# Attention visits in a fused matmul stream: TensorE's waits gathered at the head of each visit

## The chip, the cores and the metric

The kernel runs on one core of a Trainium2 chip. The metric is the time of one execution on the device in microseconds (us). Before the change it is 863.22 us, the median of three runs from 862.84 to 863.50 us.

## What is computed

A gated linear attention over 4 batches, 8 heads, 768 tokens and 48 channels per head, followed by two dense two-layer blocks over the 3072 tokens (model width 384, hidden width 2048). Cut to what matters:

```python
for t in range(S):
    state = alpha[:, :, t, :, None] * state + np.einsum('bhd,bhe->bhde', k[:, :, t], v[:, :, t])
    y[:, :, t] = np.einsum('bhd,bhde->bhe', q[:, :, t], state)
x = np.ascontiguousarray(y.transpose(0, 2, 1, 3)).reshape(B * S, H * D)
h = x @ w_in;   x = (h * np.clip(h + 3.0, 0.0, 6.0) / 6.0) @ w_out      # first block
h = x @ w_in2;  out = np.maximum(h, 0.0) ** 2 @ w_out2                  # second block
```

## The kernel before

**Steps.** TensorE's program is one list of 192 steps and two more to drain. Step g computes one slice of 128 hidden channels for 512 tokens: `hidden(g)` (L1027) is 9 matmuls of 128x512, and `project(g - 2)` (L1040) is 9 matmuls that use the slice of two steps earlier. Both split each fp32 operand into a high and a low part, so three products are summed. In between, ScalarE makes the gate (L572) and rounds the high part (L580), VectorE multiplies (L761), and GpSimd (POOL) subtracts to get the low part (`low(g)`, L499). Steps 0 to 95 are the first dense block, 96 to 191 the second.

**Attention.** The first 128 tokens of each batch (tiles 0 to 3) are done before step 0. The rest is cut into 20 tiles, 4 to 23, one tile being 64 tokens of two batches. Their TensorE work is put between the steps, in a **visit** per tile. A visit for tile t comes after the two matmul groups of its step and consists of

1. `carry_straight(t)` (L921): 8 small matmuls (L916) of the state with the queries, after its waits;
2. `attend(t)` (L960): 16 small matmuls (L969) of masked scores with values;
3. for t from 5 to 22, `add_up(t - 1)` (L986): 16 small matmuls (L995) of keys with values, for the state;
4. for t from 8 to 22, `score_later(t + 1)` (L883): 16 small matmuls (L900) of keys with queries of the **next** tile;
5. `carry_crossed(t)` (L930): 8 more matmuls (L916) of state with queries.

The profile counts each small matmul as two. From tile 9 on, the scores of a tile are thus made in the visit of the tile before (`with_output` is true); I call the visits of tiles 8 to 22 the **15 fused visits**. For tiles 4 to 8 the score is made by itself one or more steps ahead of the tile's own visit. The steps of the visits stand in `ATTEND_AT` and `LATER_ATTEND_AT`: steps 4, 7, 10, 13 of the first sixteen, then 1, 5, 9, 13 of each sixteen.

**What feeds a visit.** For a tile, VectorE scans the decays (L676, L684), and then POOL multiplies the keys (L489, `scale_keys`) and the queries (L494, `scale_queries`) by them. The semaphore `q_scaled` counts finished query scalings. In POOL's program this pair stands right behind `low(g)` of the step g that `scaled_at` names; for tiles 9 to 23 that is the step just before the fused visit in which they are scored. SyncE loads values (`v_loaded`) and, by way of device memory, the turned keys (L401, `keys_loaded`). VectorE masks the scores (`masked`) and multiplies the state (`state_decayed`), and the vector and scalar engines take the output y out of PSUM (`x_hi`, `x_lo`). TensorE itself counts `attended` after a visit's `attend`, `u_made` after `add_up`, and `y_made` after `carry_crossed`.

Of the kernel before, what the change touches and what calls it, by code (L numbers as in the profile page):

```python
# [12 lines left out]
BATCH, HEADS, SEQ, HD = 4, 8, 768, 48  # L13
# [9 lines left out]
TILES = CHUNKS * BATCH  # L23
# [46 lines left out]
LAST_SUMMED = TILES - 3  # L70
# [14 lines left out]
def slot_of(t):  # L85

    return t if t < BATCH else BATCH + t % 2


def turn_of(t):  # L90

    return 1 if t < BATCH else (t - BATCH) // 2 + 1
# [13 lines left out]
def with_output(t):  # L106

    return t - BATCH >= len(FIRST_SCORE_AT)
# [14 lines left out]
def tiles_at(g, step_of):  # L123
    return [t for t in range(BATCH, TILES) if step_of(t) == g]


def hi_parts(t):


    return t + 1 if t < BATCH - 1 else BATCH - 1 + KT + 2 * (t - BATCH + 1)  # L130


def pieces_of(t):

    return 2 * (t + 1) if t < BATCH else 2 * BATCH + t - BATCH + 1
# [22 lines left out]
def chunked_program(nc, block, semaphores, att_in, v_first, v_in, w_in1, w_out1, w_in2, w_out2, out, out_of_range,  # L158
# [4 lines left out]
    with ExitStack() as ctx:  # L163
# [12 lines left out]
        def sem(name):  # L176
            return semaphores.enter_context(nc.semaphore(name))
# [67 lines left out]
        def keys(t):  # L245
            return pairs(slot(t)[0:ROWS, 0:PAIRS * TILE])

        def queries(t):
            return pairs(slot(t)[0:ROWS, PAIRS * TILE:KQ_W])

        def values(t):
            return inputs[:, t % 2, SLOT_W:SLOT_W + DM]
# [11 lines left out]
        def side_of(j, parity):  # L264

            return parity ^ j % 2
# [31 lines left out]
        def half_rows(half):  # L298
            return slice(HALF * half, HALF * half + HD)
# [14 lines left out]
        v_loaded = [sem(f"v_loaded{i}") for i in range(BATCH + 2)]  # L314
# [9 lines left out]
        k_scaled = sem("k_scaled")  # L324
        q_scaled = sem("q_scaled")
# [5 lines left out]
        masked = sem("masked")  # L331
        blocks_turned = sem("blocks_turned")
        turned_stored = sem("turned_stored")
        keys_loaded = sem("keys_loaded")
# [6 lines left out]
        x_hi = sem("x_hi")  # L341
        x_lo = sem("x_lo")
# [14 lines left out]
        def wait_loaded(engine, semaphores, t):  # L357
            engine.wait_ge(semaphores[slot_of(t)], 16 * turn_of(t))
# [9 lines left out]
        def load_flag(name, engine):  # L368
            engine.wait_ge(range_judged, 3)
            flags[name] = engine.value_load(out_of_range[0:1, 0:1], min_val=0, max_val=1)  # L370
# [491 lines left out]
        def _(pe):  # L862
# [18 lines left out]
                                last.then_inc(scored, 1)  # L881

            def score_later(t):  # L883
                pe.wait_ge(k_scaled, t + 1)
                pe.wait_ge(q_scaled, t + 1)
                pe.wait_ge(masked, pieces_of(t - 1))
                if with_output(t):
                    pe.wait_ge(attended, t - BATCH)
                else:
                    pe.wait_ge(y_made, t)  # L890
                    pe.wait_ge(x_hi, hi_parts(t - 1))
                    pe.wait_ge(x_lo, hi_parts(t - 1))
                    pe.wait_ge(state_made, pieces_of(max(t - 2, BATCH - 1)))
                for j in range(PAIRS):
                    for b in range(2):
                        cols = slice(PART * b, PART * (b + 1))
                        for parity in range(2):
                            rows = half_rows(parity)
                            place = SCORE_COLS[parity] + j * PART
                            last = nc.tensor.matmul(att_all[cols, place:place + PART], keys(t)[rows, j, cols],  # L900
                                                    queries(t)[rows, j, cols], start=parity == 0 or not with_output(t),
                                                    stop=True, skip_group_check=True)
                last.then_inc(scored, 1)

            def carry_on(t, crossed):

                for j in range(0, PAIRS, 2):
                    for side in range(2):  # L910
                        for parity in range(2):
                            batch = parity ^ crossed
                            pair = j + (parity ^ side)
                            rows = half_rows(parity)
                            place = OUTPUT_COLS[batch] + pair * PART
                            last = nc.tensor.matmul(att_all[half_rows(side), place:place + PART],  # L916
                                                    state[rows, t % 2 * 2 + batch, pair, :],
                                                    queries(t)[rows, pair, PART * batch:PART * (batch + 1)],
                                                    start=not crossed and j == 0, stop=True, skip_group_check=True)
                return last  # L920

            def carry_straight(t):

                pe.wait_ge(state_decayed, t - BATCH + 1)
                pe.wait_ge(masked, pieces_of(t))
                pe.wait_ge(q_scaled, t + 1)
                pe.wait_ge(x_hi, hi_parts(t - 1))
                pe.wait_ge(x_lo, hi_parts(t - 1))
                carry_on(t, 0)

            def carry_crossed(t):
                pe.wait_ge(attended, t - BATCH + 1)
                if BATCH < t <= LAST_SUMMED + 1:
                    pe.wait_ge(u_made, t)
                carry_on(t, 1).then_inc(y_made, 1)
# [22 lines left out]
                last.then_inc(y_made, 1)  # L958

            def attend(t):  # L960
                wait_loaded(pe, v_loaded, t)
                pe.wait_ge(masked, pieces_of(t))
                for j in range(PAIRS):
                    for parity in range(2):
                        head = 2 * j + parity
                        for b in range(2):
                            tokens = slice(PART * b, PART * (b + 1))
                            place = OUTPUT_COLS[b] + j * PART
                            last = nc.tensor.matmul(att_all[half_rows(side_of(j, parity)), place:place + PART],  # L969
                                                    values(t)[tokens, head * HD:(head + 1) * HD], masked_part[tokens, parity, j, :],  # L970
                                                    start=False, stop=True, skip_group_check=True)
                last.then_inc(attended, 1)
# [11 lines left out]
                last.then_inc(u_made, 1)  # L984

            def add_up(t):  # L986
                pe.wait_ge(keys_loaded, 16 * (t - BATCH + 1))
                wait_loaded(pe, v_loaded, t)
                for j in range(PAIRS):
                    for parity in range(2):  # L990
                        head = 2 * j + parity
                        for b in range(2):
                            tokens = slice(PART * b, PART * (b + 1))
                            place = SUM_COLS[b] + j * HD
                            last = nc.tensor.matmul(att_all[half_rows(parity), place:place + HD],  # L995
                                                    k_tok[tokens, j, HD * parity:HD * (parity + 1)],
                                                    values(t)[tokens, head * HD:(head + 1) * HD], start=b == 0, stop=True,
                                                    skip_group_check=True)
                last.then_inc(u_made, 1)
# [86 lines left out]
            for g in range(2 * STEPS + LAG):  # L1086
                if g < 2 * STEPS:
                    hidden(g)
                if g >= LAG:
                    project(g - LAG)  # L1090
                for t in tiles_at(g, attend_at):
                    carry_straight(t)
                    attend(t)
                    if BATCH < t <= LAST_SUMMED + 1:
                        add_up(t - 1)
                for t in tiles_at(g, score_at):
                    score_later(t)
                for t in tiles_at(g, attend_at):
                    carry_crossed(t)
                if g == 2 * STEPS + LAG - 1:  # L1100
                    load_flag("pe", pe)
                if g == STEPS - FT + 8:
                    pe.wait_ge(range_judged, 2)
                    nc.tensor.matmul(att_ps[0][0:1, 0:1], in_range_all, causal[0:ROWS, TILE - 1:TILE], start=True, stop=True).then_inc(range_counted, 1)
# [290 lines left out]
```

## Time and profile before

| | |
|---|---|
| Median of three runs | 863.22 us |
| The profiled execution, as timed | 862.91 us |
| Its span in the profile | 861.2 us |
| TensorE matmul busy in the span | 853.0 us (99%) |
| VectorE, ScalarE, POOL busy | 38%, 38%, 37% |
| TensorE's granted clock, mean | 0.999 |

The profiled execution is 0.31 us below the median of the runs. The page's busy lines and the chain of waits tell which engine sets the time. The rows of the timeline give start and length of a merged group of instructions. Matmuls are pipelined, so consecutive groups overlap in the timeline: a group's length runs to the end of its last matmul, and the start of that last matmul is the group's end less the length of a single one.

### The profile page before, as it was taken

To read this page: it belongs to the slowest core of one execution; us is meant where nothing else is said; L and a number is where in the kernel's file an instruction comes from. 1 tells how busy PE (TensorE), PEld (TensorE's weight loads), DVE (VectorE), ACT (ScalarE), POOL (GpSimd) and SP (SyncE) were. 2 spreads that over 40 slices of the span, in tenths; PEclk is the share of its full clock that TensorE was granted. 3 is DMA by queue.
4 is the path that set the end of the run, shared out by engine and by line. 5 is a ranking of instruction groups with operands and counts; after the bars stand their busy time and mean duration, and the time that the engine had idled before them with its cause. 6 is when DMAs were issued, how large, how long until landed. Compare 5 with 4: busy or idle time off the path is not lost.

```text
span 861.2 us, 15383 instructions
## 1 busy us (share of the span) xinstructions
PE 853.0 (99%) x6312; PEld 705.5 (82%) x6312; DVE 330.7 (38%) x466; ACT 328.8 (38%) x586; POOL 315.3 (37%) x248
## 2 busy tenths in 40 slices
PE   8999999999999999999999999999999999999998
PEld 7877788888888888888888888888888888888886
DVE  8886545565445556422334312211211211211111
ACT  4754443343333333333454423333333323333332
POOL 2754443433443334432333333333323333333332
PEclk9999999999999999999999999999999999999999
DMA  9633323233223332200323000000000100100101
GB/s 351 260 105 92 79 72 108 73 89 79 71 71 95 85 89 76 64 16 6 108 76 111 1 0 21 17 1 8 29 1 0 37 1 1 37 0 1 37 1 38
DMA packets 67495, 51.84 MB, mean 60 GB/s; under 512 B 50784, under 2 KB 57184, under 8 KB 67424
## 3 DMA queue, kind: packets, MB, share of 16 engines
q1 hardware_dynamic: 67424, 50.84, 19.3%
q8 instruction: 51, 0.84, 0.4%
q14 instruction: 20, 0.16, 0.1%
HBM read 40.60 MB, written 8.26 MB: 57 GB/s over the span
## 4 chain that ended last, share of the span: by engine, by line
PE 96%; DMA 1%; issue 1%; ACT 0%; SPq 0%; POOL 0%; DVE 0%; ACTq 0%; DVEq 0%
PE h_ps L1027 46%; PE o_ps L1040 45%; PE att_all L916 1%; PE att_all L900 1%; DMA w_in_raw<-w_in 1%; PE att_all L969 1%; PE att_all L995 1%; SPq L379 0%; PE h_ps L953 0%; POOL g_parts L499 0%; DVE inputs L676 0%; POOL inputs L494 0%; POOL inputs L489 0%; ACT k_tok L538 0%; DVE x_mid L715 0%
## 5 line engine op out<-in xcount | busy, mean ns | idle before, releaser
L499 POOL TENSOR_TENSOR g_parts<-h_act,g_parts 128x512 fp32r<-128x512 f32 x192 | 257.0, 1339 | 523.9 <-ACT g_parts L580 523.9
L1040 PE MATMUL o_ps<-g_parts,w_out_hi 128*128 128x512 f32 x1152 | 327.1, 389 | 0.0
L1027 PE MATMUL h_ps<-x_parts,w_in_hi 128*128 128x512 f32 x1152 | 295.9, 392 | 0.0
L1040 PEld LDWEIGHTS o_ps<-g_parts,w_out_hi 128*128 128x128 f32 x1152 | 216.3, 188 | 45.0
L1027 PEld LDWEIGHTS h_ps<-x_parts,w_in_hi 128*128 128x128 f32 x1152 | 214.2, 188 | 45.3
L580 ACT ACTIVATE g_parts<-h_act 128x512 fp32r<-128x512 f32 x192 | 121.4, 632 | 268.2 <-PE o_ps L1040 241.9
L764 DVE SCALAR_TENSOR_TENSOR h_act<-h_ps,h_gate 128x512 f32<-128x512 f32 x96 | 66.4, 691 | 290.5 <-ACT h_gate L575 290.5
L1040 PE MATMUL o_ps<-g_parts,w_out_lo 128*128 128x512 f32 x576 | 165.6, 389 | 0.0
L1027 PE MATMUL h_ps<-x_parts,w_in_lo 128*128 128x512 f32 x576 | 161.9, 389 | 0.0
L1027 PEld LDWEIGHTS h_ps<-x_parts,w_in_lo 128*128 128x128 f32 x576 | 108.1, 188 | 22.7
L1040 PEld LDWEIGHTS o_ps<-g_parts,w_out_lo 128*128 128x128 f32 x576 | 108.1, 188 | 22.4
L761 DVE SCALAR_TENSOR_TENSOR h_act<-h_gate,h_ps 128x512 f32<-128x512 f32 x96 | 65.4, 681 | 139.7 <-ACT h_gate L572 139.6
L572 ACT ACTIVATE h_gate<-h_ps 128x512 f32<-128x512 f32 x96 | 57.4, 598 | 116.6 <-PE h_ps L1027 116.5
L575 ACT ACTIVATE h_gate<-h_ps 128x512 f32<-128x512 f32 x96 | 57.4, 598 | 110.8 <-PE h_ps L1027 110.8
L684 DVE TENSOR_TENSOR_SCAN inputs<-inputs,seeds 112x520 f32<-112x520 f32 x20 | 37.4, 1872 | 0.7
L742 DVE TENSOR_TENSOR tails<-att_all,tails 112x128 fp32r<-112x128 f32 x20 | 5.9, 293 | 57.8 <-ACT x_parts L559 57.8
L676 DVE TENSOR_TENSOR_SCAN inputs<-inputs,seeds 112x520 f32<-112x520 f32 x20 | 25.6, 1280 | 2.5 <-DVE seeds L673 0.5
L494 POOL TENSOR_TENSOR inputs<-inputs 112x512 f32<-112x512 f32 x20 | 24.5, 1226 | 0.0
L489 POOL TENSOR_TENSOR inputs<-inputs 112x512 f32<-112x512 f32 x20 | 23.9, 1196 | 0.0
L715 DVE STREAM_TRANSPOSE x_mid<-inputs 128x512 f32<-128x512 f32 x18 | 19.7, 1092 | 0.0
L916 PEld LDWEIGHTS att_all<-inputs,state 48*48 48x48 f32 x640 | 12.5, 120 | 8.4 <-issue 7.9
L916 PE MATMUL att_all<-inputs,state 48*48 48x64 f32 x640 | 17.5, 222 | 0.8 <-PE att_all L995 0.6
(107 smaller groups left out, 357.8 us busy)
## 6 DMA issues: line engine op xcount, KB each, us to landing
inputs<-att_in SPq DMA_DIRECT2D x20, 772.0 KB, 4.5
w_in_raw<-w_in SPq DMA_DIRECT2D x8, 768.0 KB, 7.7
w_out_raw<-w_out SPq DMA_DIRECT2D x8, 768.0 KB, 9.2
result<-inputs SPq DMA_DIRECT2D x18, 256.0 KB, 2.3
inputs<-v_in SPq DMA_DIRECT2D x20, 192.0 KB, 2.8
k_tok<-turned_keys SPq DMA_DIRECT2D x18, 192.0 KB, 2.9
turned_keys<-x_mid SPq DMA_DIRECT2D x36, 64.0 KB, 2.3
x_parts<-tails SPq DMA_DIRECT2D x120, 16.0 KB, 2.1
```

Of the source, the lines that this page charges most:

```text
L494: nc.gpsimd.tensor_tensor(by_chunk(t, queries(t)), by_chunk(t, queries(t)), to_token(t)[:, :, 0:chunk(t)], ALU.mult).then_inc(q_scaled, 1)
L499: nc.gpsimd.tensor_tensor(g_parts[:, g % 2, 1, :], h_act[:, g % 2, :], g_parts[:, g % 2, 0, :].bitcast(F32), ALU.subtract).then_inc(g_lo, 1)
L572: nc.scalar.activation(h_gate[:, g % 2, :], h_ps[g % 2][:, :], ACT.Relu, bias=0.5, scale=1.0 / 6.0).then_inc(gate_made, 1)
L575: nc.scalar.activation(h_gate[:, g % 2, :], h_ps[g % 2][:, :], ACT.Relu).then_inc(gate_made, 1)
L580: nc.scalar.activation(g_parts[:, g % 2, 0, :], h_act[:, g % 2, :], ACT.Copy).then_inc(g_hi, 1)
L676: nc.vector.tensor_tensor_scan(scanned(t, ATT_W), scanned(t, KQ_W), other_seeds(t), 0.0, ALU.mult, ALU.max).then_inc(from_end_made, 1)
L684: nc.vector.tensor_tensor_scan(loaded[:, ::-1], loaded[:, ::-1], other_seeds(t), 0.0, ALU.mult, ALU.max).then_inc(to_token_made, 1)
L761: nc.vector.scalar_tensor_tensor(h_act[:, g % 2, :], h_gate[:, g % 2, :], 1.0, h_ps[g % 2][:, :], ALU.min, ALU.mult).then_inc(act_made, 1)
L764: nc.vector.scalar_tensor_tensor(h_act[:, g % 2, :], h_ps[g % 2][:, :], 0.0, h_gate[:, g % 2, :], ALU.max, ALU.mult).then_inc(act_made, 1)
L916: last = nc.tensor.matmul(att_all[half_rows(side), place:place + PART], state[rows, t % 2 * 2 + batch, pair, :], queries(t)[rows, pair, PA ...
L1027: last = nc.tensor.matmul(h_ps[g % 2][:, :], w[:, m, cols], x_parts[:, n % 2, part, m, :], start=m == 0 and i == 0, stop=m == KT - 1 and i ...
L1040: return nc.tensor.matmul(o_ps[m][:, :], w[:, f, m * P:(m + 1) * P], g_parts[:, g % 2, part, :], start=f == 0 and w is w_out_hi and part = ...
```

## The change

Four functions of TensorE's program change; no computation, buffer or transfer does, and no other engine's program does.

- `wait_for_visit(t)` takes the place of the waits of `carry_straight(t)`. It waits for `state_decayed` and `masked` as before, no longer for `q_scaled` of its own tile, `x_hi` and `x_lo`, and in addition for `v_loaded`, for `keys_loaded` (where an `add_up` follows) and, where a `score_later(t + 1)` follows in the visit, for `q_scaled` of tile t + 1.
- `attend` and `add_up` have no waits of their own any more.
- `score_later(t)` no longer waits for `k_scaled` and `masked`; in the fused visits it waits for `attended` alone. Standing alone (tiles 4 to 8) it keeps `q_scaled`, `y_made`, `x_hi`, `x_lo` and `state_made`.
- `carry_crossed` keeps its waits for `attended` and `u_made`.

```diff
             def score_later(t):
-                pe.wait_ge(k_scaled, t + 1)
-                pe.wait_ge(q_scaled, t + 1)
-                pe.wait_ge(masked, pieces_of(t - 1))
+
                 if with_output(t):
                     pe.wait_ge(attended, t - BATCH)
                 else:
+                    pe.wait_ge(q_scaled, t + 1)
                     pe.wait_ge(y_made, t)
...
-            def carry_straight(t):
+            def wait_for_visit(t):
+
 
                 pe.wait_ge(state_decayed, t - BATCH + 1)
                 pe.wait_ge(masked, pieces_of(t))
-                pe.wait_ge(q_scaled, t + 1)
-                pe.wait_ge(x_hi, hi_parts(t - 1))
-                pe.wait_ge(x_lo, hi_parts(t - 1))
-                carry_on(t, 0)
+                wait_loaded(pe, v_loaded, t)
+                if BATCH < t <= LAST_SUMMED + 1:
+                    pe.wait_ge(keys_loaded, 16 * (t - BATCH))
+                if t + 1 < TILES and with_output(t + 1):
+                    pe.wait_ge(q_scaled, t + 2)
...
             def attend(t):
-                wait_loaded(pe, v_loaded, t)
-                pe.wait_ge(masked, pieces_of(t))
...
             def add_up(t):
-                pe.wait_ge(keys_loaded, 16 * (t - BATCH + 1))
-                wait_loaded(pe, v_loaded, t)
...
                 for t in tiles_at(g, attend_at):
-                    carry_straight(t)
+                    wait_for_visit(t)
+                    carry_on(t, 0)
                     attend(t)
```

The first place is TensorE's program at the first fused visit, that of tile 8. In brackets stand the semaphores for which an instruction waits, with `L` the line that issues it. Before:

```order
L916 MATMUL att_all<-inputs,state 48x64 [waits x_hi,q_scaled,x_lo,masked,state_decayed]
L916 MATMUL att_all<-inputs,state 48x64 x7
L969 MATMUL att_all<-masked_t,inputs 48x64 [waits masked,v_loaded4]
L969 MATMUL att_all<-masked_t,inputs 48x64 x15
L995 MATMUL att_all<-inputs,k_tok 48x48 [waits v_loaded5,keys_loaded]
L995 MATMUL att_all<-inputs,k_tok 48x48 x15
L900 MATMUL att_all<-inputs 64x64 [waits masked,attended,q_scaled,k_scaled]
L900 MATMUL att_all<-inputs 64x64 x15
L916 MATMUL att_all<-inputs,state 48x64 [waits u_made,attended]
```

The same visit after the change (line numbers differ by up to 3):

```order
L915 MATMUL att_all<-inputs,state 48x64 [waits keys_loaded,v_loaded4,q_scaled,masked,state_decayed]
L915 MATMUL att_all<-inputs,state 48x64 x7
L968 MATMUL att_all<-masked_t,inputs 48x64 x16
L992 MATMUL att_all<-inputs,k_tok 48x48 x16
L899 MATMUL att_all<-inputs 64x64 [waits attended]
L899 MATMUL att_all<-inputs 64x64 x15
L915 MATMUL att_all<-inputs,state 48x64 [waits u_made,attended]
```

No matmul moved. The wait for the next tile's `q_scaled` stood in front of the fourth group and now stands in front of the first; of the ten waits inside the visit three are left (`attended` twice and `u_made`), and the head has five as before.

The second place is TensorE's program at the visit of tile 5, which has no score in it. Before:

```order
L916 MATMUL att_all<-inputs,state 48x64 [waits x_hi,q_scaled,x_lo,masked,state_decayed]
L916 MATMUL att_all<-inputs,state 48x64 x7
L969 MATMUL att_all<-masked_t,inputs 48x64 [waits masked,v_loaded5]
L969 MATMUL att_all<-masked_t,inputs 48x64 x15
L995 MATMUL att_all<-inputs,k_tok 48x48 [waits v_loaded4,keys_loaded]
L995 MATMUL att_all<-inputs,k_tok 48x48 x15
L916 MATMUL att_all<-inputs,state 48x64 [waits u_made,attended]
```

After the change:

```order
L915 MATMUL att_all<-inputs,state 48x64 [waits v_loaded5,keys_loaded,masked,state_decayed]
L915 MATMUL att_all<-inputs,state 48x64 x7
L968 MATMUL att_all<-masked_t,inputs 48x64 x16
L992 MATMUL att_all<-inputs,k_tok 48x48 x16
L915 MATMUL att_all<-inputs,state 48x64 [waits u_made,attended]
```

Here the two loads are waited for at the head, and `q_scaled` not at all. POOL's program is the same before and after.

## Rows read from the trace of the kernel before

**Rows 1.** The page: header, busy time by engine, granted clock, chain by line.

```profile
span 861.2 us, 15383 instructions
...
PE 853.0 (99%) x6312; PEld 705.5 (82%) x6312; DVE 330.7 (38%) x466; ACT 328.8 (38%) x586; POOL 315.3 (37%) x248
...
PEclk9999999999999999999999999999999999999999
```

**Rows 2.** Waits of TensorE: engine, line, releaser: us in total, times, longest us.

```profile
PE h_ps L865 <- POOL causal L472: 2.0, 1, 2.0
PE o_ps L953 <- DVE h_gate L722: 0.7, 1, 0.7
PE att_all L916 <- PE att_all L995: 0.6, 3, 0.2
...
PE att_all L983 <- ACT k_tok L538: 0.3, 1, 0.3
```

**Rows 3.** Timeline, PE, fused visit of tile 9: start us, length us, instructions merged.

```profile
125.45 0.84 PE L1040 MATMUL o_ps<-g_parts,w_out_hi 128*128 128x512 f32 x3
126.22 0.44 PE L916 MATMUL att_all<-inputs,state 48*48 48x64 f32 x16
126.49 0.63 PE L969 MATMUL att_all<-masked_t,inputs 64*48 64x64 f32 x32
126.93 0.54 PE L995 MATMUL att_all<-inputs,k_tok 64*48 64x48 f32 x32
127.41 0.69 PE L900 MATMUL att_all<-inputs 48*64 48x64 f32 x32
127.90 0.43 PE L916 MATMUL att_all<-inputs,state 48*48 48x64 f32 x16
```

**Rows 4.** Groups by line, PE: busy us, mean ns of one, idle before.

```profile
L969 PE MATMUL att_all<-masked_t,inputs 64*48 64x64 f32 x640 | 12.6, 216 | 0.0
L995 PE MATMUL att_all<-inputs,k_tok 64*48 64x48 f32 x576 | 9.7, 205 | 0.0
```

**Rows 5.** Timeline, PE, fused visit of tile 8.

```profile
107.44 0.44 PE L916 MATMUL att_all<-inputs,state 48*48 48x64 f32 x16
...
108.16 0.54 PE L995 MATMUL att_all<-inputs,k_tok 64*48 64x48 f32 x32
108.79 0.69 PE L900 MATMUL att_all<-inputs 48*64 48x64 f32 x32
```

**Rows 6.** Timeline, PE, fused visit of tile 22, the last.

```profile
367.58 0.44 PE L916 MATMUL att_all<-inputs,state 48*48 48x64 f32 x16
...
368.29 0.54 PE L995 MATMUL att_all<-inputs,k_tok 64*48 64x48 f32 x32
368.74 0.69 PE L900 MATMUL att_all<-inputs 48*64 48x64 f32 x32
```

**Rows 7.** Timeline, POOL, around the visit of tile 9.

```profile
123.02 1.29 POOL L499 TENSOR_TENSOR g_parts<-h_act,g_parts 128x512 fp32r<-128x512 f32 x1 [1.60 <-ACT g_parts L580]
124.27 1.19 POOL L489 TENSOR_TENSOR inputs<-inputs 112x512 f32<-112x512 f32 x1
125.42 1.19 POOL L494 TENSOR_TENSOR inputs<-inputs 112x512 f32<-112x512 f32 x1
127.10 1.27 POOL L499 TENSOR_TENSOR g_parts<-h_act,g_parts 128x512 fp32r<-128x512 f32 x1 [0.49 <-ACT g_parts L580]
```

**Rows 8.** Timeline, POOL, query scaling around the visit of tile 8.

```profile
107.50 1.19 POOL L494 TENSOR_TENSOR inputs<-inputs 112x512 f32<-112x512 f32 x1
```

**Rows 9.** Timeline, POOL, around the visit of tile 22.

```profile
364.38 1.29 POOL L499 TENSOR_TENSOR g_parts<-h_act,g_parts 128x512 fp32r<-128x512 f32 x1 [2.79 <-ACT g_parts L580]
...
366.77 1.20 POOL L494 TENSOR_TENSOR inputs<-inputs 112x512 f32<-112x512 f32 x1
```

**Rows 10.** Timeline, PE, the visit of tile 4: no add_up and no score in it.

```profile
43.53 0.63 PE L969 MATMUL att_all<-masked_t,inputs 64*48 64x64 f32 x32
44.27 0.44 PE L916 MATMUL att_all<-inputs,state 48*48 48x64 f32 x16
```

**Rows 11.** Timeline, SyncE's queue: a load of keys (L401), one of values (L389).

```profile
51.72 0.57 SPq L401 DMA_DIRECT2D k_tok<-turned_keys  x1
...
66.93 0.62 SPq L389 DMA_DIRECT2D inputs<-v_in  x1
```

**Rows 12.** The page, DMA issues: instructions, KB each, median us from issue to landing.

```profile
inputs<-v_in SPq DMA_DIRECT2D x20, 192.0 KB, 2.8
...
k_tok<-turned_keys SPq DMA_DIRECT2D x18, 192.0 KB, 2.9
```

**Rows 13.** Timeline, PE, first group of the visits of tiles 5 and 6.

```profile
57.97 0.44 PE L916 MATMUL att_all<-inputs,state 48*48 48x64 f32 x16
...
73.08 0.44 PE L916 MATMUL att_all<-inputs,state 48*48 48x64 f32 x16
```

**Rows 14.** Busy table of 12 to 20 us: us, busy PE, PEld, DVE, ACT, POOL, PEclk.

```profile
12.00:20.00 8.00, 7.34 (x159) 6.68 (x155) 7.64 (x13) 5.24 (x12) 1.19 (x1) 1.00 1.03 410
```

**Rows 15.** Timeline, PE, in that stretch: in brackets the idle time before and its releaser.

```profile
16.41 1.53 PE L953 MATMUL o_ps<-h_gate,first_v 128*64 128x128 f32 x24 [0.66 <-DVE h_gate L722]
```

**Rows 16.** The chain that ended last: one group of each kind in a step.

```profile
345.00 2.04 PE h_ps L1027 x9
347.04 2.04 PE o_ps L1040 x9
```

## Prediction

> **What bounds the kernel now.** I read the page first. TensorE is busy 99% of the span and the other compute engines under 40% each, at a granted clock near full in every slice [rows 1]. So whatever TensorE waits for at one place is added to the time, and whatever it saves comes off it. The view of waits then says that TensorE hardly waits for anybody: five small rows near the start and in the first block, and none that names `x_hi`, `x_lo`, `k_scaled`, values or loaded keys in a visit [rows 2]. Taking waits away can therefore give back only the cost of passing a wait that is already satisfied, and for that one has to look at the seams between groups in the timeline.
>
> The timeline of a fused visit shows the seams [rows 3]. The start of a group's last matmul is its end less one matmul, 0.216 us for L969 and 0.205 us for L995 [rows 4]. L969 ends at 126.49 + 0.63 = 127.12, so its last matmul starts at 126.90, and L995 follows at 126.93: a seam of 0.03 us. L995's last matmul starts at 126.93 + 0.54 - 0.205 = 127.27, and L900, the score, starts at 127.41: a seam of 0.14 us. The last seam, L900 to L916, has L916 start at 127.90 while L900 ends at 128.10, an overlap of a whole matmul. Only the seam in front of the score, with its four waits, costs anything.
>
> The third thing to read is when the awaited events happen. The one that matters is the scaling of the next tile's queries on POOL, because its wait moves from the fourth group to the first. For tile 9's visit POOL's L494 ends at 125.42 + 1.19 = 126.61 [rows 7], but the visit starts at 126.22 and its score at 127.41 [rows 3]. **The scaling ends inside the visit**: soon enough for where the wait stands now, and 0.39 us too late for the head.
>
> **The change part by part.**
>
> *The moved wait, 14 visits.* In tile 22's visit it is the same: L494 ends at 366.77 + 1.20 = 367.97 [rows 9], the head is at 367.58 [rows 6], 0.39 us. These are the first and the last of 14 visits (tiles 9 to 22) with L494 ending 0.38 to 0.40 us behind the head. To this comes the time from POOL's end to TensorE's first matmul. Tile 8 shows it: there L494 ends at 107.50 + 1.19 = 108.69 [rows 8] and the score starts at 108.79 [rows 5], and its other releasers are long done, so 0.10 us. Each of the 14 heads moves back by 0.39 + 0.10 = 0.49 us: 14 x 0.49 = 6.86 us.
>
> *The moved wait, tile 8.* The head is at 107.44 [rows 5] and could now start at 108.79: 1.35 us.
>
> *Do the delays catch up?* I say no. POOL's pair of scalings stands directly behind `low(g)`, and that one starts when ScalarE delivers, 1.60 us after POOL ran dry at tile 9 and 2.79 us at tile 22 [rows 7, 9]. ScalarE is fed by TensorE's hidden matmuls of that step. So when TensorE is late by some time, POOL's scaling is late by the same, and the next head is again 0.39 us too early. Nothing else stands between TensorE's groups that could shrink.
>
> *Waits taken out in front of the score, 15 visits.* The seam there is 0.14 us at tile 9 and 368.74 - (368.29 + 0.54 - 0.205) = 0.115 us at tile 22 [rows 6], between 0.11 and 0.14 us in all 14. At tile 8 it is 108.79 - (108.16 + 0.54 - 0.205) = 0.295 us, since `q_scaled` came late [rows 5]. I take 0.035 us, the neighbouring seam of L969 to L995, for what is left. Is `attended`, still waited for there, in the way? Tile 4's visit has no `add_up` between: L969's last matmul starts at 43.53 + 0.63 - 0.216 = 43.94 and the dependent L916 at 44.27 [rows 10], so the event needs 0.33 us. In a fused visit `add_up` fills 0.37 us of that and more [rows 3], so it is hidden with about 0.07 us to spare. Saving: 0.26 us at tile 8 and on the mean 0.08 us in the other 14, 1.15 us, together 1.4 us. The bounds are nothing and, were the seams to close as L900 to L916 does, 0.4 us more.
>
> The Trainium skill's page "TensorE: Matmul & The Clock Gate" (Part 1, Architectural detail) gives TensorE a queue 64 deep. By that the sequencer would have passed the score's waits far ahead, nothing would be saved there, and the sum would be 1.4 us higher. The seam of 0.14 us beside one of 0.03 us speaks against it [rows 3], so the trace's value stays in the sum; the page's case is the third rival.
>
> *Waits taken out elsewhere.* `masked` and `v_loaded` in front of L969, `v_loaded` and `keys_loaded` in front of L995: the seams there are already 0.03 us [rows 3], so nothing comes back. `x_hi`, `x_lo` and its own `q_scaled` at the head: no row of the waits names them [rows 2], and the head's five waits stay five, so nothing. The bound from the trace is the score's seam, 0.08 us a visit, if they cost what its waits cost; the five that stay make me leave that out.
>
> *Loads waited for earlier.* `keys_loaded` and `v_loaded` come forward by under 0.8 us. The first key load is issued at 51.72 [rows 11] and lands 2.9 us later [rows 12], at 54.6, against a head at 57.97 [rows 13]. The first values loaded in turn are issued at 66.93 and land at 69.7, against a head at 73.08 [rows 13]. That is over 3 us to spare in the tightest place; 0. What hides them is the distance of four steps; if it were gone, each would cost its lateness as the scaling does.
>
> *Visits of tiles 4 to 7 and 23, scores standing alone:* same seams, 0. The seam for `u_made` at tiles 5 to 7 stays. What waits behind TensorE's head is only TensorE's own next step, and the engines that wait for a visit (VectorE's state update, ScalarE's rounding) get it later with four steps until the next.
>
> **Sum:** 6.86 + 1.35 - 1.41 = 6.8 us. The profiled execution becomes 862.91 + 6.8 = 869.7 us; its median lies 0.31 us above, 863.22 + 6.8 = **870.0 us**, 0.8% slower.
>
> **Rivals.**
>
> *Faster: the head's wait is hidden.* POOL's spans are rough by the page's own account, and if the semaphore rose over 0.4 us before L494's recorded end, the head would wait for nothing and only the saving would be left: 863.22 - 1.4 = 861.8 us. It decides at a lateness that equals the saving, 0.08 us a visit. Against it: at tile 8 the score started just 0.10 us after that end, with nothing else to wait for. 3%.
>
> *No change: the delay is caught up.* If POOL ran on a beat of its own, one delay would cure the next visit's, and only tile 8's 1.35 us less 1.4 us would remain: 863.2 us. Against it: POOL idle behind ScalarE before each pair [rows 7, 9]. 3%.
>
> *Slower still, nothing saved in front of the score:* 6.86 + 1.35 = 8.2 us, 871.4 us. For it: `attended` is still waited for. 8%.
>
> *Slower still, the clock falls.* TensorE stood idle for 0.66 us at 16.41 and the granted clock stayed at 1.00 over that stretch, the 2.4 GHz level [rows 14, 15]; tile 8's gap would be 1.35 us. A step is two groups of 9 matmuls at 2.04 us each [rows 16], 4.1 us; one at the 1.2 GHz level costs 4.1 us more, 874 us. 2%.
>
> **How the numbers follow.** The forecast has 84%; its own range is the lateness of 0.38 to 0.40 us, a releaser's time of 0.07 to 0.13 us, a saving from 0.5 to 1.8 us: 14 x 0.45 + 1.32 - 1.8 = 5.8 us to 14 x 0.53 + 1.38 - 0.5 = 8.3 us, or 869.0 to 871.5. That takes in the third rival's 871.4. The runs before spread by 0.3 us to either side, which I add below: 868.7 to 871.5 us. Outside are the first two rivals, the falling clock and a few in a hundred of the forecast's own. A measurement of this kernel can tell 0.2% (1.7 us) from no change. Faster by more than that: 0.02; within: 0.04; slower: 0.94.
>
> **What would show it.** In the new profile the head's L915 should start 0.10 us behind the end of POOL's L494 in every fused visit and TensorE should be listed as waiting for POOL 15 times, some 0.4 to 0.5 us each and 1.3 us once. The seam L992 to L899 should be 0.03 to 0.04 us. The visits of tiles 4 to 7 and 23 should be as before. The prediction is wrong if L494 shifts against the head, if the head does not wait for it, or if the score's seam stays.

## The result, and the profile after

| | before | after the change |
|---|---|---|
| Median | 862.88 us (6 runs, 862.80 to 863.50) | 870.06 us (6 runs, 869.28 to 870.77) |
| Profiled execution, as timed | 862.91 us | 870.47 us |
| Its span | 861.2 us | 868.8 us |

The ratio of the times is 1.0081, with a 95% interval from 1.0070 to 1.0092: slower by 0.8%, 7.2 us between the medians. The forecast was 870.0 us.

The chain of work that ended last now runs through POOL for a part of the time. Its shares by engine, before and after:

```profile
PE 96%; DMA 1%; issue 1%; ACT 0%; SPq 0%; POOL 0%; DVE 0%; ACTq 0%; DVEq 0%
```

```profile
PE 89%; POOL 6%; ACT 2%; DMA 1%; issue 1%; SPq 0%; DVE 0%; ACTq 0%; DVEq 0%
```

The view of waits of TensorE has a new first row (engine, line, releaser: us in total, times, longest us). It answers to [rows 2].

```profile
PE att_all L915 <- POOL inputs L494: 7.8, 15, 1.3
PE h_ps L865 <- POOL causal L472: 2.0, 1, 2.0
PE o_ps L954 <- DVE h_gate L722: 0.7, 1, 0.7
```

TensorE waits for POOL's query scaling 15 times, once in each fused visit, and the longest of them is tile 8's. The timeline of TensorE around tile 9's visit answers to [rows 3] (start us, length us, instructions merged, in brackets the idle time before and its releaser).

```profile
127.05 0.84 PE L1037 MATMUL o_ps<-g_parts,w_out_hi 128*128 128x512 f32 x3
128.36 0.44 PE L915 MATMUL att_all<-inputs,state 48*48 48x64 f32 x16 [0.46 <-POOL inputs L494]
128.59 0.66 PE L968 MATMUL att_all<-masked_t,inputs 64*48 64x64 f32 x32
129.04 0.56 PE L992 MATMUL att_all<-inputs,k_tok 64*48 64x48 f32 x31
129.39 0.23 PE L899 MATMUL att_all<-inputs 48*64 48x64 f32 x1
...
129.43 0.65 PE L899 MATMUL att_all<-inputs 48*64 48x64 f32 x31
129.87 0.43 PE L915 MATMUL att_all<-inputs,state 48*48 48x64 f32 x16
130.24 1.66 PE L1024 MATMUL h_ps<-x_parts,w_in_hi 128*128 128x512 f32 x6
```

The row of the kernel before to compare the last one with:

```profile
128.26 1.65 PE L1027 MATMUL h_ps<-x_parts,w_in_hi 128*128 128x512 f32 x6
```

Before, the head came 126.22 - 125.45 = 0.77 us behind the start of the last three large matmuls; now it is 128.36 - 127.05 = 1.31 us, 0.54 us later. From the head to the next step's first matmul it was 2.04 us (126.22 to 128.26) and is 1.88 us (128.36 to 130.24), 0.16 us less. Net 0.38 us here. (Tile 9's seam before was a bit wide; in the other visits the net is 0.39 to 0.43 us, but for tile 12's, 0.78 us, with a pause behind it.)

POOL around the same visit, answering to [rows 7]:

```profile
124.62 1.29 POOL L499 TENSOR_TENSOR g_parts<-h_act,g_parts 128x512 fp32r<-128x512 f32 x1 [1.60 <-ACT g_parts L580]
...
127.01 1.20 POOL L494 TENSOR_TENSOR inputs<-inputs 112x512 f32<-112x512 f32 x1
```

POOL's idle time in front of `low(g)` is 1.60 us as before. L494 starts 125.42 - 125.45 = 0.03 us ahead of the large group L1040 in the old trace and 127.01 - 127.05 = 0.04 us ahead of it in the new: POOL has moved with TensorE, and each head is again too early by the same amount. At tile 22 the same holds, after the delays of tiles 8 to 21, with 2.79 us of idle time as in [rows 9]:

```profile
371.59 1.29 POOL L499 TENSOR_TENSOR g_parts<-h_act,g_parts 128x512 fp32r<-128x512 f32 x1 [2.79 <-ACT g_parts L580]
...
373.99 1.20 POOL L494 TENSOR_TENSOR inputs<-inputs 112x512 f32<-112x512 f32 x1
```

And tile 8's visit, answering to [rows 5]:

```profile
107.68 0.39 PE L1037 MATMUL o_ps<-g_parts,w_out_hi 128*128 128x512 f32 x1
109.39 0.44 PE L915 MATMUL att_all<-inputs,state 48*48 48x64 f32 x16 [1.33 <-POOL inputs L494]
```

The visits without a score did not change their shape. Behind tile 12's visit the new trace also has a pause with no releaser, which I come back to at the end (PEld is TensorE's weight loads):

```profile
188.88 0.19 PEld L1024 LDWEIGHTS h_ps<-x_parts,w_in_lo 128*128 128x128 f32 x1 [0.52 <-issue]
```

### The profile page after: what moved, and what is told of

Its sections match the earlier page's. It is cut to its first block, busy times and chain, and to the rows that moved or that the text cites. A ratio compares the mean times of both kernels' runs of the same rounds, so it can differ in the third digit from the quotient of the medians.

```text
span 868.8 us, 15308 instructions
## 1 busy us (share of the span) xinstructions
PE 852.1 (98%) x6312; PEld 703.6 (81%) x6312; DVE 330.2 (38%) x466; ACT 328.5 (38%) x586; POOL 315.0 (36%) x248
## 4 chain that ended last, share of the span: by engine, by line
PE 89%; POOL 6%; ACT 2%; DMA 1%; issue 1%; SPq 0%; DVE 0%; ACTq 0%; DVEq 0%
PE h_ps L1024 42%; PE o_ps L1037 41%; POOL g_parts L499 2%; POOL inputs L494 2%; POOL inputs L489 2%; PE att_all L915 2%; DMA w_in_raw<-w_in 1%; PE att_all L899 1%; ACT g_parts L580 1%; PE att_all L968 1%; PE att_all L992 1%; SPq L379 0%; PE h_ps L954 0%; DVE inputs L676 0%; ACT k_tok L538 0%
## 5 line engine op out<-in xcount | busy, mean ns | idle before, releaser
L494 POOL TENSOR_TENSOR inputs<-inputs 112x512 f32<-112x512 f32 x20 | 24.5, 1226 | 0.0
```

What stands on the lines that cost most here:

```text
L494: nc.gpsimd.tensor_tensor(by_chunk(t, queries(t)), by_chunk(t, queries(t)), to_token(t)[:, :, 0:chunk(t)], ALU.mult).then_inc(q_scaled, 1)
```

## The experiments

The medians below are of 11 runs of each kernel, but for the moved wait alone (4 runs) and the two with another order of the waits (5 each). The kernel before ran beside them: its median was 863.15 us beside the first four kernels (27 runs) and 863.01 us beside the last four (21 runs). The seams of single visits are worked out from the rows shown, which are rounded to 0.01 us.

### The moved wait alone

```diff
                 pe.wait_ge(x_lo, hi_parts(t - 1))
+                if t + 1 < TILES and with_output(t + 1):
+                    pe.wait_ge(q_scaled, t + 2)
                 carry_on(t, 0)
```

> The kernel before, with one wait added: in the 15 fused visits the head also waits for q_scaled of the next tile. All other waits stay. My theory (the moved wait is the whole loss): each of 14 heads moves back to 0.10 to 0.15 us behind the end of POOL's L494, 0.49 to 0.53 us later than now, and tile 8's 1.35 us, while the score's seam keeps its 0.11 us and loses 0.18 us at tile 8: 14 x 0.51 + 1.35 - 0.18 = 8.3 us more than before, about 871.2 us, and 1 us above the changed kernel. Rival (the removed waits or a changed instruction stream cost something as well): clearly under 869 us.

Measured: 872.02 us, ratio 1.0101 (1.0085 to 1.0116), 8.9 us over the kernel before. TensorE's waits, and tile 9's visit in the timeline:

```profile
PE att_all L916 <- POOL inputs L494: 8.0, 15, 1.3
```

```profile
127.12 0.84 PE L1042 MATMUL o_ps<-g_parts,w_out_hi 128*128 128x512 f32 x3
128.44 0.44 PE L916 MATMUL att_all<-inputs,state 48*48 48x64 f32 x16 [0.47 <-POOL inputs L494]
...
129.12 0.56 PE L997 MATMUL att_all<-inputs,k_tok 64*48 64x48 f32 x32
129.59 0.69 PE L900 MATMUL att_all<-inputs 48*64 48x64 f32 x32
```

The head is at 128.44, 1.32 us behind the large group, and the seam of the score is still there: L997's last matmul starts at 129.12 + 0.56 - 0.205 = 129.475 and L900 at 129.59, 0.115 us later. One added wait brings more than the whole loss, and the other edits of the change take 1.7 us of it back (8.9 against 7.2 us, each over the kernel before in its own set of runs). The median is 0.8 us over what I expected. The trace has two reasons: each of the 14 heads is 0.546 us later, not 0.51, 0.5 us in sum, and four visits of this profile have a wider seam in front of the score (0.18 to 0.27 us, 0.4 us in sum), such as tile 11's. What widens them was not tried.


```profile
167.32 0.56 PE L997 MATMUL att_all<-inputs,k_tok 64*48 64x48 f32 x32
167.95 0.69 PE L900 MATMUL att_all<-inputs 48*64 48x64 f32 x32
```

### All but the moved wait

```diff
                 if with_output(t):
+                    pe.wait_ge(q_scaled, t + 1)
                     pe.wait_ge(attended, t - BATCH)
...
-                if t + 1 < TILES and with_output(t + 1):
-                    pe.wait_ge(q_scaled, t + 2)
```

> The changed kernel with q_scaled of the next tile waited for in front of the score again, beside attended, instead of at the head; values, keys, masked gathered at the head as in the change. My theory: the heads start as before, and the score's seam of 0.11 to 0.14 us shrinks to about 0.03 us, but tile 8's 0.30 us stays since q_scaled comes late there: 14 x 0.08 = 1.1 us less than before, about 861.8 us. Rival (one separate wait instruction in front of the score is enough to make the seam, however many stand there): the seam stays at 0.11 us and the time within 0.3 us of before, 862.9 us.

Measured: 861.88 us, ratio 0.9989 (0.9980 to 0.9998), 1.3 us under the kernel before. Tile 9's visit:

```profile
125.41 0.84 PE L1036 MATMUL o_ps<-g_parts,w_out_hi 128*128 128x512 f32 x3
126.19 0.44 PE L916 MATMUL att_all<-inputs,state 48*48 48x64 f32 x16
...
126.89 0.54 PE L991 MATMUL att_all<-inputs,k_tok 64*48 64x48 f32 x32
127.27 0.69 PE L900 MATMUL att_all<-inputs 48*64 48x64 f32 x32
```

The head stands 0.78 us behind the large group, as before, and the seam is 127.27 - (126.89 + 0.54 - 0.205) = 0.045 us. So the change without the moved wait is a small gain, and the rival (one separate wait is enough for the seam) is out.

### The changed kernel, with the scaling a step earlier

```diff
 def decays_at(t):
-    return score_at(t) - (2 if with_output(t) else 3)
+    return score_at(t) - 3
...
 def scaled_at(t):
-    return 0 if t == BATCH else score_at(t) - (1 if with_output(t) else 2)
+    return 0 if t == BATCH else score_at(t) - 2
```

> The changed kernel, and for tiles 9 to 23 VectorE's decays and POOL's scaling of keys and queries are done one step (4.1 us) earlier in their programs. My theory: the head's wait for q_scaled is then satisfied some 3.7 us ahead, so the whole loss of 6.9 + 1.35 us is gone and the savings stay, seams of 0.03 us or less in front of the score: 1.4 to 1.9 us under before, 861.0 to 861.5 us, faster than both kernels. Rival (gathered waits at the head cost by their number, not by lateness): over 863 us. Rival (POOL's pair in the earlier step makes low() late for project()): TensorE waits for g_parts L499 and the time is over 863 us.

Measured: 861.10 us, ratio 0.9977 (0.9968 to 0.9986), 2.0 us under the kernel before and 9 us under the changed one. POOL and TensorE around tile 9's visit:

```profile
124.90 1.19 POOL L494 TENSOR_TENSOR inputs<-inputs 112x512 f32<-112x512 f32 x1
126.05 1.28 POOL L499 TENSOR_TENSOR g_parts<-h_act,g_parts 128x512 fp32r<-128x512 f32 x1
```

```profile
127.86 0.84 PE L1037 MATMUL o_ps<-g_parts,w_out_hi 128*128 128x512 f32 x3
128.63 0.44 PE L915 MATMUL att_all<-inputs,state 48*48 48x64 f32 x16
...
129.34 0.54 PE L992 MATMUL att_all<-inputs,k_tok 64*48 64x48 f32 x32
129.70 0.66 PE L899 MATMUL att_all<-inputs 48*64 48x64 f32 x32
...
130.51 1.66 PE L1024 MATMUL h_ps<-x_parts,w_in_hi 128*128 128x512 f32 x6
```

The same five waits stand at the head. L494 ends at 126.09, 2.5 us ahead of it (I expected 3.7 us; it is enough), the head is 0.77 us behind the large group and the seam is 0.025 us. The number of waits at the head is not what costs; their lateness is. No row of TensorE's waits names `g_parts` or POOL's L494.

The profiled execution is the slowest of the 11 runs, 863.57 us, 2.5 us over their median. Its extra time lies ahead of the visits: the group of tile 4 starts at 46.02 us, against 43.1 to 43.9 us in the other nine profiles, and one wait near the start is 1.5 us long:

```profile
PE o_ps L982 <- ACT k_tok L538: 1.5, 1, 1.5
```

The fused visits are undisturbed.

### The control: the kernel before, with the scaling a step earlier

The same edit of the two functions, in the kernel before.

> The control: the kernel before with the same decays and scalings one step earlier. My theory: only tile 8's seam of 0.30 us falls to 0.11 us, 862.7 us, within 0.3 us of before; so what the run with the changed waits gains over this one is the waits' own worth. Rival (the earlier scaling helps by itself, whatever the waits): as fast as the run of the changed kernel with early scaling.

Measured: 863.17 us, ratio 1.0000 (0.9991 to 1.0009). The earlier scaling by itself brings nothing that the median shows. In the trace it closes tile 8's wide seam from 0.30 to 0.11 us, as expected:

```profile
108.04 0.54 PE L995 MATMUL att_all<-inputs,k_tok 64*48 64x48 f32 x32
108.48 0.69 PE L900 MATMUL att_all<-inputs 48*64 48x64 f32 x32
```

Against this control the run above is 2.1 us faster, and the two kernels differ in TensorE's waits alone.

### The wait written first

```diff
             def wait_for_visit(t):
+                if t + 1 < TILES and with_output(t + 1):
+                    pe.wait_ge(q_scaled, t + 2)
                 pe.wait_ge(state_decayed, t - BATCH + 1)
...
-                if t + 1 < TILES and with_output(t + 1):
-                    pe.wait_ge(q_scaled, t + 2)
```

> The changed kernel with the head's wait for the next tile's q_scaled written first of the five instead of last, so that the head's first matmul carries it itself and not a separate wait instruction. In the changed kernel the head starts 0.145 us behind POOL's end. My theory (0.05 us of that is a separate wait instruction that begins only once its first condition holds): the head starts 0.08 us behind POOL's end, as tile 4's L916 did behind attended, 15 x 0.06 = 0.9 us less than the changed kernel, about 869.2 us. Rival (the lag is the semaphore's way and does not depend on which instruction waits): 0.145 us as now and 870.1 us.

Measured: 868.26 us, ratio 1.0066 (1.0052 to 1.0080), 1.8 us under the changed kernel where I expected 0.9. Around tile 9:

```profile
127.80 0.44 PE L915 MATMUL att_all<-inputs,state 48*48 48x64 f32 x16 [0.36 <-POOL inputs L494]
```

```profile
126.56 1.19 POOL L494 TENSOR_TENSOR inputs<-inputs 112x512 f32<-112x512 f32 x1
```

L494 ends at 127.75 and the head starts at 127.80: 0.05 us, where in the changed kernel it is 128.36 - 128.21 = 0.15 us. Without rounding it is 0.054 against 0.145 us. Over the 15 visits the heads come 1.4 us earlier against the large matmuls than in the changed kernel's profile; the pause behind tile 12's visit, 0.4 us, is not in this profile either. Together that is the 1.8 us. The rival (the lag does not depend on which instruction waits) is out.

### The wait as second condition of its pair

The five waits of the head in the order `state_decayed`, `q_scaled`, `v_loaded`, `keys_loaded`, `masked`.

> The changed kernel with the five waits of the head in another order, so that q_scaled is the second condition of the separate wait instruction whose first is masked, as it was in front of the score before. My theory: the instruction begins on masked, long satisfied, and is done when POOL's end comes, so the head starts 0.10 us behind POOL's end, as tile 8's score did in the kernel before, instead of 0.145 us: 15 x 0.045 = 0.7 us less than the changed kernel, about 869.4 us. Rival (the order of the two conditions means nothing): 0.145 us and 870.1 us.

Measured: 869.77 us, ratio 1.0080 (1.0066 to 1.0093), runs from 869.11 to 870.59. Around tile 9:

```profile
127.58 0.44 PE L915 MATMUL att_all<-inputs,state 48*48 48x64 f32 x16 [0.42 <-issue]
```

```profile
126.28 1.20 POOL L494 TENSOR_TENSOR inputs<-inputs 112x512 f32<-112x512 f32 x1
```

L494 ends at 127.48, the head starts 0.10 us later, so the lag did shrink by 0.045 us a visit as expected, and the 15 heads together come 0.7 us earlier than in the changed kernel's profile. The median moved by 0.3 us instead of 0.7, within the spread of this kernel's runs; the time alone would not tell. The separate wait instructions can be asked for by their line (name, times, shortest/median/longest in ns, first and last start). Here, and in the changed kernel:

```profile
L930 PEldq EVENT_SEMAPHORE  x20: 51/4470/5308, 39.8 to 388.4; - x20
```

```profile
L930 PEldq EVENT_SEMAPHORE  x15: 51/51/51, 109.3 to 375.2; - x15
```

In this run the instruction begins early, on `masked`, and lasts 4.4 to 5.3 us in the fused visits, until 0.044 us behind POOL's end. In the changed kernel, with `q_scaled` as its first condition, it begins only 0.04 us behind POOL's end, takes 0.05 us and ends 0.09 us behind it. The difference of 0.045 us is that of the lags, so the theory is shown.

### One wait less in front of the score

```diff
             def score_later(t):
                 pe.wait_ge(k_scaled, t + 1)
                 pe.wait_ge(q_scaled, t + 1)
-                pe.wait_ge(masked, pieces_of(t - 1))
```

> The kernel before with only the wait for masked taken from score_later: in a fused visit its first matmul carries k_scaled, and one separate wait instruction (attended, q_scaled) is left in front of it where there were two. Nothing else changes. My theory (the seam is the second of two wait instructions in a row, which the queued matmuls no longer cover): the seam in front of the score falls from 0.11 to 0.04 us in 14 visits and from 0.30 to 0.27 us at tile 8, 1.1 us less, about 862.0 us, as good as gathering all of them. Rival (the seam comes from the waits inside attend and add_up, which use up the lead): the seam stays over 0.08 us and the time within 0.4 us of before, 863.1 us.

Measured: 861.96 us, ratio 0.9986 (0.9977 to 0.9995), 1.05 us under the kernel before. Tile 9:

```profile
126.75 0.54 PE L994 MATMUL att_all<-inputs,k_tok 64*48 64x48 f32 x32
127.12 0.69 PE L899 MATMUL att_all<-inputs 48*64 48x64 f32 x32
```

The seam is 127.12 - (126.75 + 0.54 - 0.205) = 0.035 us. Tile 8's seam stays at 0.30 us, where I expected 0.27. This one line gives nearly all that the change without the moved wait gives (1.3 us), and about half of the 2.1 us that the change gives over its control once the scaling is early. The separate wait instructions in front of the score are two in the kernel before:

```profile
L886 PEldq EVENT_SEMAPHORE  x15: 51/51/51, 108.4 to 368.5; - x15
L888 PEldq EVENT_SEMAPHORE  x15: 51/51/240, 108.5 to 368.6; - x15
```

Here one is left:

```profile
L887 PEldq EVENT_SEMAPHORE  x15: 51/51/310, 108.3 to 367.3; - x15
```

### The gathering, with the score's four waits kept

The waits of `attend` and `add_up` gathered at the head and `q_scaled`, `x_hi`, `x_lo` dropped there; `score_later` as before.

> The kernel before with the waits of attend and add_up gathered at the head, and the superfluous ones there gone, as the change does, but with the score's four waits (k_scaled, q_scaled, masked, attended) left where they are. My theory: two wait instructions still stand in front of the score, the seam there stays at 0.11 us and tile 8's at 0.30 us, 863.1 us, no change. Rival (the lead lost inside attend and add_up makes the seam): the seam falls to 0.04 us or so and the time to about 862 us.

Measured: 863.12 us, ratio 1.0000 (0.9991 to 1.0009). Tile 9:

```profile
126.80 0.54 PE L991 MATMUL att_all<-inputs,k_tok 64*48 64x48 f32 x32
127.25 0.69 PE L900 MATMUL att_all<-inputs 48*64 48x64 f32 x32
```

The seam is still 0.115 us. The waits inside `attend` and `add_up` and the superfluous ones at the head cost nothing where they were; those in front of the score did.

The seam is only a part of what they cost. The whole is seen from the head's first matmul to the first matmul of the next step, as the mean over the visits of tiles 9 to 22 of each profile:

| Separate wait instructions in front of the score | Kernels | Head to next step, us |
|---|---|---|
| two | before; before with early scaling; the score's four waits kept | 2.01 |
| two, with four wider seams | the moved wait alone | 2.04 |
| one | all but the moved wait; the score without `masked` | 1.93 |
| none (`attended` alone, on the first weight load) | changed; changed with early scaling; both with another order at the head | 1.88 |

All ten kernels fall into these rows, whether their head waited for POOL or not. So the second instruction costs 0.08 us a visit, which is the seam that shrank, and the last one another 0.05 us, of which the seam shows a third where the head was not held up (0.04 to 0.025 us).

## Why the prediction was right

The forecast of 870.0 us met 870.06 us, and its mechanism was the right one. That the numbers agree to 0.1 us is luck: two terms were too small by 0.7 us each and cancelled, and two smaller differences of 0.3 to 0.4 us did so too (item 7).

1. **What bounds the kernel.** Right. The row of waits shows 7.8 us of idle time. The heads moved by more, 8.9 us in sum against the large matmuls in front of them, since each had overlapped the end of the last large one by 0.07 us, and the row counts only idle time. From this comes off what the waits in front of the score gave back.
2. **The moved wait, 14 visits.** The mechanism was right, and shown by the added wait alone (8.9 us) and by its disappearance once the scaling is early (861.10 us). The term was too small: I took 0.10 us from POOL's end to the head, from tile 8's score, and it is 0.145 us. Each head moved by 0.535 us instead of 0.49, 7.5 us instead of 6.86. The two runs with another order of the waits show why tile 8's row did not carry over: the lag depends on where the wait is written, 0.05, 0.10 or 0.15 us, and in front of tile 8's score `q_scaled` was the second condition of its instruction.
3. **Tile 8.** Forecast 1.35 - 0.26 = 1.09 us. The whole stretch, from the start of the last large matmul ahead of the visit to that of the last in the hidden group behind it, grew from 4.49 to 5.55 us, 1.06 us. Here too both parts were somewhat larger: the head moved by 1.40 us, and 0.31 us came back.
4. **Delays do not catch up.** Right: POOL's idle time ahead of its pair is unchanged to the hundredth at tiles 9 and 22.
5. **What was saved.** Too small: 1.41 us was forecast, 2.1 us came, which is even above the 1.8 us that I gave as bound. At a typical visit it is 0.125 us from head to next step (2.005 to 1.88), where I took 0.08. I read the cost of the waits off the seam alone, and took the neighbouring seam of 0.035 us for what is left; the table above shows that the last separate instruction costs 0.05 us more, most of it outside that seam. The third rival (nothing saved) is out. The head's first group takes 0.03 us less to the second when a separate wait instruction has held it up (0.23 against 0.26 us), but this is no part of the saving: the run with the moved wait alone has it and saves nothing behind its head, and the run with the wait written first lacks it and has the full saving.
6. **Waits elsewhere at nothing.** Right for those of `attend`, `add_up` and the superfluous ones at the head, shown by the run that gathers them and keeps the score's four (ratio 1.0000), and the earlier wait for loads too, which that run has as well.
7. **The sum.** Net of a visit: forecast 0.49 - 0.08 = 0.41 us, measured 0.38 to 0.43 us. In sum over the 15 visits the heads moved by 8.9 us and 2.1 us came back, which leaves the 6.8 us forecast. The stretches as in item 3 took 64.4 us before and 71.5 us after in the two profiles, 7.1 us more; 0.4 us of that is the pause behind tile 12, which nothing in the prediction foresaw. The two medians differ by 7.2 us, 0.4 us more than forecast, and this does not show in 870.06 us because the kernel before came out at 862.88 us over six runs, 0.34 us under the median from which the forecast starts.
8. **The rivals.** The hidden wait and the caught-up delay would have shown fewer waits for POOL. The clock did not fall: its mean was 1.000.
9. **The signs.** The 15 waits for POOL came, 0.46 us at a typical visit and 1.3 us once. The head was to start 0.10 us behind L494 and starts 0.145 us behind it. The seam in front of the score was to be 0.03 to 0.04 us, and the score's first matmul now starts even before `add_up`'s last (129.39 us, with 31 of the 32 matmuls of L992 merged in the row above it).

Where I weighed the queue depth of 64 that the Trainium skill's "TensorE: Matmul & The Clock Gate" (Part 1, Architectural detail) gives, the runs say that a queue of this depth does not by itself hide satisfied waits: with two separate wait instructions in front of the score a seam of 0.11 us stays, with one it is 0.04 us. The Trainium skill's "Perfetto Trace Analysis" (Identifying Dependency Chains) says that instructions which wait for several engines may have EventSemaphore instructions inserted ahead of them for the additional conditions. The traces agree: they list these instructions, two, one or none in front of the score. That their number sets the time of a visit agrees with all ten profiles; why the second shows in the seam and the last hardly does is not shown.

## What to carry to other kernels

Before a wait is moved to the head of a block, look in the timeline for the end of its releaser. If that lies inside the block, expect the bound engine to pay the difference each time; and if the producer is fed by the same engine, do not count on it to catch up: here it did not in any of the 15 visits. Gathering waits was worth something only in front of the score, where several satisfied ones stood together; for `attend` and `add_up` it brought nothing. It also needs the releasers ahead of the head: moving the scaling one step (nothing by itself) turned a loss of 7.2 us into a gain of 2.0 us. So count the separate wait instructions in front of a group of short matmuls, and where one wait is known to end last, write it first: that alone took 0.09 us off each head here.

## What was not expected

- The lag from the releaser's end to the first waiting matmul depended on the place of the wait in the list: 0.05 us when written first, 0.10 us as second condition of a separate wait instruction, 0.15 us as its first.
- The profiles of the changed kernel and of the one with the wait second of its pair both have a pause without a releaser behind tile 12's visit (0.52 and 0.50 us), in which TensorE's weight loads stand still; none of the other eight has it. The packed traces hold a clue. In these two a transfer of 16 KB of instructions starts 2.0 us before the pause begins (at 186.36 and 185.43 us) and is the first in 18 us; each of the other eight has one more such transfer in the same stretch (at 181.06 us in the run with the wait first). A load of TensorE's program that comes too late would fit this. Which engine the transfers are for cannot be read from the traces, and it was not tried, so the cause stays open.
- The times of the changed kernel and of the one with the wait second spread over 1.5 us, while four of the five runs with the wait first lie within 0.2 us, and the fifth is 1.7 us higher. Whether the pause comes and goes between runs is not known, since one execution of each kernel was profiled.
